# Two inner loops for the tensor engine, products of constants ahead of the first keys, and an earlier split of z, in a squared-ReLU attention with a mixture of experts

## The reference, cut to what matters

```
scores = (1/S) * z z^T                 S = 3072
attn   = max(scores, 0)^2
x      = u * (attn v)
```

## Time and profile before

| | |
|---|---|
| median of 3 runs | 934.61 us (933.88 to 936.75) |
| the profiled execution, own time | 933.74 us |
| its span, first to last instruction | 932.0 us |
| PE busy | 889.1 us (95%) |
| DVE, ACT, POOL busy | 641.1, 611.7, 120.8 us |
| mean granted clock of PE | 0.99 |
| group 0 of the attention | about 23.6 to 59.4 us |
| the loop over groups | to 648.1 us |
| the experts | from 656.5 us |

### The profile page before, as it was taken

How to read it: one execution, slowest core, us unless ns; L and a number is a source line. 1 busy time by engine, 2 the same in 40 slices (tenths; PEclk the granted TensorE clock), 3 DMA queues, 4 the chain that set the end, 5 groups by cost and what they waited for, 6 DMA issues and landing times.

```text
span 932.0 us, 23370 instructions
## 1 busy us (share of the span) xinstructions
PE 889.1 (95%) x7695; PEld 707.2 (76%) x7696; DVE 641.1 (69%) x1377; ACT 611.7 (66%) x927; POOL 120.8 (13%) x120
## 2 busy tenths in 40 slices
PE   3999899999999999999999999998799999999995
PEld 1787787888888888888888888886577777777774
DVE  6876767877877888788787787666264655566430
ACT  6877686777787779887778787786245434434531
POOL 0001101101101110110110110011012121211212
PEclk9999999999999999999999999999799999999998
DMA  9964519513522740010010004200414224313100
GB/s 266 207 177 152 170 35 314 169 59 110 169 99 70 225 138 14 31 34 17 17 34 17 17 32 116 79 23 20 159 35 155 89 79 152 130 52 134 51 17 34
DMA packets 85575, 90.78 MB, mean 97 GB/s; under 512 B 15677, under 2 KB 80394, under 8 KB 85552
## 3 DMA queue, kind: packets, MB, share of 16 engines
q1 hardware_dynamic: 80656, 77.84, 27.9%
q0 software_dynamic: 4896, 12.64, 3.8%
HBM read 46.33 MB, written 44.93 MB: 98 GB/s over the span
## 4 chain that ended last, share of the span: by engine, by line
PE 86%; DVE 5%; issue 3%; DMA 2%; ACT 1%; POOLq 1%; SPq 0%; POOL 0%; DVEq 0%; ACTq 0%
PE Sc L752 14%; PE O L626 13%; PE O L630 13%; PE O L628 13%; PE Sc L604 7%; PE Sc L605 7%; PE O L773 5%; PE O L775 5%; PE O L777 4%; PE M L675 1%; DMA rawv<-in_v 1%; PE M L730 1%; DMA disp<-xrow,slot 1%; DVE attn_hi L904 1%; PE M L580 1%
## 5 line engine op out<-in xcount | busy, mean ns | idle before, releaser
L626 PE MATMUL O<-vS,attn_hi 128*128 128x256 f16 x1332 | 363.5, 273 | 0.6 <-DVE ubuf L954 0.6
L628 PE MATMUL O<-vS,attn_hi 128*128 128x256 f16 x1332 | 363.6, 273 | 0.0
L630 PE MATMUL O<-vS,attn_lo 128*128 128x256 f16 x1332 | 363.5, 273 | 0.0
L426 ACT ACTIVATE Sc<-Sc 128x768 f32<-128x768 f32 x224 | 178.5, 797 | 76.3 <-PE Sc L605 65.7
L910 DVE TENSOR_TENSOR attn_lo<-attn,attn_hi 128x768 f16<-128x768 f32 x224 | 214.7, 958 | 7.7
L430 ACT ACTIVATE attn<-Sc 128x768 f32<-128x768 f32 x224 | 181.7, 811 | 7.1
L604 PE MATMUL Sc<-zP 128*128 (+1 forms) x450 | 148.0, 329 | 6.8 <-ACT attn L430 3.0
L904 DVE CAST attn_hi<-attn 128x768 f16<-128x768 f32 x224 | 125.1, 558 | 39.8 <-ACT attn L430 28.7
L626 PEld LDWEIGHTS O<-vS,attn_hi 128*128 128x128 f16 x1332 | 130.4, 98 | 26.7 <-DVE ubuf L954 1.0
L628 PEld LDWEIGHTS O<-vS,attn_hi 128*128 128x128 f16 x1332 | 130.4, 98 | 25.5 <-issue 0.2
L605 PE MATMUL Sc<-zQ,zP 128*128 (+1 forms) x450 | 148.1, 330 | 0.0
(11 more groups left out here) (141 smaller groups left out, 879.5 us busy)
## 6 DMA issues: line engine op xcount, KB each, us to landing
out<-empty SPq DMA_DIRECT2D x8, 3072.0 KB
wraw<-in_moe_w SPq DMA_DIRECT2D x16, 1024.0 KB
rawv<-in_v SPq DMA_DIRECT2D x16, 768.0 KB, 9.1
ubuf<-in_u SPq DMA_DIRECT2D x19, 384.0 KB, 3.2
disp<-empty SPq DMA_DIRECT2D x8, 774.0 KB, 17.1
vS<-disp SPq DMA_DIRECT2D x16, 387.0 KB, 3.3
rawz<-in_z SPq DMA_DIRECT2D x3, 768.0 KB
disp<-xrow,slot POOLq DMA_INDIRECT x54
```

Source lines behind the costliest of these rows:

```text
L426: act.activation(pair, pair, ACT.Relu).then_inc(s["relu_done"], 1)
L626: nc.tensor.matmul(o_part(t), hi, v[:, 0:D], start=c == 0 and j == 0 and t % 2 == 0, stop=False, skip_group_check=True)
L628: nc.tensor.matmul(o_part(t), hi, v[:, D:2 * D], start=False, stop=False, skip_group_check=True)
L630: ins = nc.tensor.matmul(o_part(t), lo, v[:, 0:D], start=False, stop=c == PAIRS - 1 and j == 1, skip_group_check=True)
```

## The change

Three parts. On PE, 60 products of constants (an identity and ones, into a part of O that nothing reads) are put ahead of the first transposes. The making of the first keys is reordered: all four slices of z are split ahead of the sums of v on DVE, all four copies to zP and zQ are made by DVE, slices 1 and 2 are transposed ahead of the scores of pairs 0 to 2, and only the transposes and the copy of slice 3 stand in group 0, at pair 2. And the loop of PE becomes an outer loop over two batches with two inner loops of a batch each, one for each value of `par`; the way out sets the inner loops' ends to 0.

```diff
 (ACT)
-            def keys_out(q):
-                act.wait_ge(s["keys_psum"], 2 * q + 2)
-                for m, dst in enumerate((zP, zQ)):
-                    act.activation(dst[:, q * SLICE * P:(q + 1) * SLICE * P],
-                                   M[m][:, :].bitcast(F16)[:, 0:SLICE * P], ACT.Copy).then_inc(s["keys_ready"], 1)
...
-                        if peeled and c // PSLICE < SLICES - 2 and c % PSLICE == 1:
-                            keys_out(c // PSLICE + 2)
 (PE)
+            def turn_over(times):
+                for _ in range(times):
+                    nc.tensor.matmul(Oa[:, 1, D:D + P], identh[:, :], ones[:, :], start=True, stop=True,
+                                     skip_group_check=True)
+            turn_over(60)
             first_keys(0)
-            pe.wait_ge(s["keys_ready"], 2)
+            first_keys(1)
             scores(0, 0, 0, 0)
             scores(1, 0, 1, 0)
-            first_keys(1)
+            first_keys(2)
             scores(2, 0, 2, 0)
...
-                        if peeled and c % PSLICE == 0 and c // PSLICE < SLICES - 2:
-                            first_keys(c // PSLICE + 2)
+                        if peeled and c == LAST_KEYS_AT:
+                            first_keys(SLICES - 1)
...
+                    for register in (stop0, stop1, stop):
+                        pe.reg_mov(register, 0)
                 both_parts(pe, n, end, part, close)
-            def either_body(n, end):
-                if isinstance(n, int):
-                    body(n, end, 0)
-                else:
-                    with pe.If((n & 8) == 0):
-                        body(n, end, 0)
-                    with pe.Else():
-                        body(n, end, 1)
-            attention_loop(pe, either_body)
+            body(0, end, 0)
+            pe.reg_mov(stop, NG + 1)
+            pe.reg_mov(low, 1)
+            with pe.Fori(0, stop, 16) as first_of_two:
+                pe.reg_mov(stop0, first_of_two + 8)
+                pe.reg_mov(stop1, first_of_two + 16)
+                with pe.If(first_of_two > NG - 1):
+                    pe.reg_mov(stop0, NG + 1)
+                    pe.reg_mov(stop1, 0)
+                with pe.Fori(low, stop0) as n:
+                    body(nc.s_assert_within(n, 1, NG), end, 0)
+                with pe.If(pe.snap(stop1) > 0):
+                    with pe.Fori(first_of_two + 8, stop1) as n:
+                        body(nc.s_assert_within(n, 8, NG - 1), end, 1)
+                pe.reg_mov(low, first_of_two + 16)
 (DVE)
             first_z(0)
             first_z(1)
             first_out(0)
+            first_z(2)
+            first_out(1)
+            first_z(3)
             dve.wait_ge(s["vparts0"], SLICES)
             dve.tensor_reduce(mx[:, 1:2], vsum[:, 0:SLICES], AX.X, ALU.add).then_inc(s["vsum0"], 1)
-            first_out(1)
...
             first_v(1)
+            first_out(2)
...
-                        if peeled and c % PSLICE == 0 and c // PSLICE < SLICES - 2:
-                            first_z(c // PSLICE + 2)
+                        if peeled and c == LAST_KEYS_AT:
+                            first_out(SLICES - 1)
 (constants)
+LAST_KEYS_AT = 2
```

More of the change, by code:

```diff
@@ L606, in scores @@
                 ins.then_inc(s["scores_ready"], 1)
+            def turn_over(times):
[3 more added lines that the diff above has]
+            turn_over(60)
             first_keys(0)
-            pe.wait_ge(s["keys_ready"], 2)
+            first_keys(1)
             scores(0, 0, 0, 0)
             scores(1, 0, 1, 0)
-            first_keys(1)
+            first_keys(2)
             scores(2, 0, 2, 0)
+            end, stop0, stop1, stop, low = (pe.alloc_register(f"pe_{name}") for name in
+                                            ("end", "stop0", "stop1", "stop", "low"))
             def body(n, end, par):
```

## The result

| | before | changed |
|---|---|---|
| median of six runs each, us | 933.67 (932.43 to 936.75) | 925.93 (923.98 to 928.73) |
| profiled execution, own time (span), us | 933.74 (932.0) | 923.98 (922.2) |
| mean granted clock of PE in it | 0.990 | 0.991 |

The ratio is 0.9915, 95% interval 0.9892 to 0.9938: 0.85% faster. The direction was right, and so were the two places where a gain was forecast, the waits of group 0 and the stall of the loop. A third, the clock at the start, had been put at nothing, and the amount was too small by 3.3 us. The profiled execution of the changed kernel is the fastest of its six, so the 9.76 us between the two profiles are more than the 7.74 us between the medians.

A forecast was written before the change was run, and what follows sets the result against it. PE was taken to bound the kernel, with 86% of the span. Keys 3.2, products 0 and loops 2.2 sum to 5.4 us: 933.7 to 928.3, plus 0.9 for the median, 929.2 us; range 926.3 to 932.0.

The forecast's parts named there:

- the waits of group 0: In group 0 PE waits twice for DVE to split a slice of z, 1.63 and 0.64 us; both were to go.
- the stall of the loop: In the loop's first turn PE stands still 2.49 us at 93.1 us, put down to one first-time jump; to go.
- the clock at the start: Up to 22.3 us: clock comes up early, falls again, rises as before; gain 0, bounds 1.9 gained to 1.0 lost.
- Keys: Group 0: PE loses two waits on DVE and one of two sets of transposes; 3.2 us gained.
- Loops: First loop turn: the jump past the par 1 body goes, 2.49 us less 0.3 for new edges; 2.2 us gained.
- (b): Loop: the stall only moves, first passage over some new edge costs the same 2.49 us; 931.4 us, chance 0.11.
- (d): Loop: slower, a stall of 2.49 us at every new edge; 938.9 us, chance 0.07.
- (c): Group 0: keys bring nothing, DVE or the loads replace the wait; only the loops count, 932.4 us, chance 0.07.
- Products: Kernel start: 60 transposes of constants from 4.4 us take 4.2 to 7.2 us; gain 0, depending on the clock at 22.3.
- (a): Kernel start: the clock stays up through it, 1.9 us more gained; 927.3 us, chance 0.13.

The follow-up runs named there:

- the one with its start bridged: Kernel before, old key order and loop, with products of constants ahead of the first keys (60) and in idle stretches up to pair 3's scores (16, 60, 20): 935.55 us.

## Why the prediction was right in direction and too small

**Keys: right.** What was said of DVE held: the split of the fourth slice starts its last step at 16.77 us and the sum over v starts at 17.31, 0.2 us after ACT's last read-out ends (16.91 + 0.19); the copy of slice 3 is done long before pair 9; there is no new wait, and at the group's end DVE still waits 2.37 us for PE. I took 3.2 us; at the clock that I assumed it is 3.40 (3.15 to 3.58 in the other executions in which the clock fell).

**Loops: right, a little small.** I took 2.2 of the 2.49 us and charged 0.3 for steps at the new edges. Measured are 2.54, and PE idles by at most 0.5 us anywhere in the loop, so the edges cost nothing that can be seen. That the sequencer's lead hides them, as I had reckoned, fits this and is not shown by itself. Rivals (b) and (d) are out, with L721 and L724 at 0.228 us and less. The Trainium skill (Runtime: NRT & Kernel Launch, "Instruction fetch mechanics") has a taken branch to a page not held pay for a fetch; the trace agrees for the first jump past a whole body, 3.38 us with a block fetched in it, and does not for the returns of the loops, old or new, which took 0.256 us or less: between 96 and 290 us, over nearly six turns, the trace of before has no instruction fetch at all.

**Rival (c) is out:** the keys came through.

**Products: right in sum.** They change nothing by the medians. In the old order with the products the clock came up at 8.7 us and fell at 18.94, ahead of the dense work, as I had forecast. What I had not seen is that it can come up without them: it rose near 18 us in three of the four profiled executions that have no products (17.75 and 18.41 us with the new keys, 18.07 with the old ones).

**The clock at the start: this step failed.** "So I take it that the clock comes up early, falls again before 22.3, and rises as before ... gain 0." It did in four of six profiled executions, and in the other two, the one profiled after the change among them, it stayed up, which is rival (a), and is worth 1.63 us by the key distance (11.78 against 13.41 us; I had 1.9). The same code goes either way. I gave the two outcomes 0.62 and 0.13 as if one of them would hold for the kernel. The six runs of the comparison have mean granted clocks from 0.984 (928.73 us, the slowest) to 0.991 (923.98 us, the fastest), so their median is taken over executions of both sorts.

**The size, added up.** The forecast was 3.27 us above the median. 0.94 is the reference: I took 934.61 from three runs, and the six of the comparison gave 933.67 (the 48 runs of the kernel before beside the experiments have medians of 933.58 to 934.43 us on three chips). 0.34 is the loops, 0.2 the keys. That leaves 1.8, which I put down to the clock; it is a remainder and was not measured by itself. Three places can hold it. At the start, up to 1.63 in the executions that keep it. At the experts' start, 1.0 between the two profiled executions, but there the difference is chance, as told above. And in the loop's stall: it did not bring the clock down in the execution profiled before, but it did in two others with the old loop. One stretch each, of the kernel before with the 60 products and of the one with its start bridged, just behind the stall:

```profile
94.10:97.40 3.30, 3.12 (x13) 2.01 (x14) 1.82 (x6) 1.60 (x3) 0.00 (x0) 0.50 0.02 5
```

```profile
96.30:99.60 3.30, 3.30 (x17) 2.27 (x16) 2.09 (x7) 2.75 (x5) 0.00 (x0) 0.50 0.00 0
```

The first loop turn then takes 37.33 and 37.55 us instead of 35.88: the stall cost 4.0 and 4.2 us in those executions, not 2.5. How the 1.8 divides among the three in the median is not settled, since of the timed runs only the profiled ones have a trace; the others have a mean clock alone. The range ended at 926.3 because (a) with 1.0 for the experts was counted from the 934.61, and did not allow for this third place. Counted from 933.67 it would have ended at 925.4, below what was measured.

## What to carry to other kernels

A clock gain counted here only where PE was not released by another engine next: with the keys late it was worth nothing, and with the keys early 1.6 us. Price a clock that can fall either way as a share of the executions and not as one outcome, and where PE is sparse ahead of dense work, put products of constants right up to that work, not at the start of the kernel: here the 60 at the start changed nothing, and 72 more up to the first weighing brought 1.7 us beside the same kernel. Then look at what moved: in the runs here, products in the instruction stream also moved the time at which the next block of instructions was fetched.

## What the runs showed of the hardware that was not expected

- The clock rose to the upper level in a stretch made of transposes and some scores alone (17.75 us without the products), and it fell or stayed in the same program from one execution to the next.
- An idle PE of 2.4 to 2.5 us in the loop brought the clock down in two of the four profiled executions of the old loop.
- One branch on PE's sequencer cost 3.28 to 3.38 us, over four executions, when first taken past a whole loop body, with a block of instructions fetched in it, and 0.26 us or less ever after.
- A scatter of POOL took 2.82 to 3.42 us instead of 2.06 in the three executions in which a block of instructions was fetched during it; which causes which was not tested.
